# Tokens pass through the experts in four groups of 384 instead of three groups of 512

## The reference

```python
# 1. chunked attention over 2 x 8 heads, 768 positions, head size 64, 8 memory keys
for c in range(24):                                  # chunks of 32 queries
    k_full = concat(mem_k, k[c*32-16 : c*32+40])     # at most 64 keys
    a = softmax(scale * q_c @ k_full.T)              # + 1e-9 in the denominator
    out[c] = a @ v_full
x = out.reshape(1536, 512)

# 2. first mixture: 4 experts, gates given
p = domain_probs / (domain_probs.sum(-1) + 1e-9)
x = sum(p[:, e:e+1] * (relu(x @ w1[e]) @ w2[e]) for e in range(4))   # 512 -> 1024 -> 512

# 3. second mixture: 8 experts, gates from the tokens
P = exp(x @ w_gate - max)
for _ in range(8):
    P /= P.sum(1); P /= P.sum(0); P *= 1536 / 8
out = sum(P[:, e:e+1] * (relu(x @ w1[e]) @ w2[e]) for e in range(8))
```

## Time and profile before

| | |
|---|---|
| time, median of 3 executions | 1686.27 us (1685.75 to 1688.09) |
| span of the profiled execution, first to last instruction | 1684.4 us |
| own time of the profiled execution | not listed apart from its span |
| PE busy | 1651.6 us, 98% of the span |
| DVE busy | 489.4 us, 29% |
| ACT busy | 322.8 us, 19% |
| POOL busy | 35.3 us, 2% |
| share of PE in the chain that ended last | 94% |

### The profile page before, as it was taken

How to read it: one execution, slowest core, us unless ns; L and a number is a source line. 1 busy time by engine, 2 the same in 40 slices (tenths; PEclk the granted TensorE clock), 3 DMA queues, 4 the chain that set the end, 5 groups by cost and what they waited for, 6 DMA issues and landing times.

```text
span 1684.4 us, 19145 instructions
## 1 busy us (share of the span) xinstructions
PE 1651.6 (98%) x8037; PEld 1363.8 (81%) x8037; DVE 489.4 (29%) x811; ACT 322.8 (19%) x551; POOL 35.3 (2%) x39
## 2 busy tenths in 40 slices
PE   6799999999999999999999999999999999999999
PEld 5778888888888887888888888888888888888887
DVE  5541321231231242272132132123123123123212
ACT  4631221121121131121121121112112112112110
POOL 2310000000000000000000000000000000000000
PEclk9799999999999999999999999999999999999999
DMA  8950020020020011002002002002002001100001
GB/s 188 147 167 1 0 100 1 1 100 0 0 99 0 0 50 51 1 3 98 1 0 100 0 0 100 0 0 100 0 0 99 0 0 59 40 0 0 8 17 50
DMA packets 50964, 66.56 MB, mean 40 GB/s; under 512 B 27880, under 2 KB 27880, under 8 KB 50928
## 3 DMA queue, kind: packets, MB, share of 16 engines
q1 hardware_dynamic: 50928, 66.04, 13.5%
HBM read 62.89 MB, written 3.15 MB: 39 GB/s over the span
## 4 chain that ended last, share of the span: by engine, by line
PE 94%; SPq 3%; issue 1%; DVE 1%; ACT 0%; DMA 0%; POOL 0%; POOLq 0%
PE banks L356 31%; PE banks L355 31%; PE banks L357 31%; SPq L187 1%; SPq L186 1%; PE banks L435 0%; DMA v_bd<-in_mem_v 0%; SPq L193 0%; SPq L189 0%; PE banks L316 0%; DVE acc L755 0%; PE banks L406 0%; PE banks L408 0%; PE banks L395 0%; SPq L169 0%
## 5 line engine op out<-in xcount | busy, mean ns | idle before, releaser
L706 DVE SCALAR_TENSOR_TENSOR h_lo<-banks,h_hi 128x512 fp32r<-128x512 f32 x288 | 199.0, 691 | 1130.0 <-ACT h_hi L571 1130.0
L356 PE MATMUL banks<-w_hi,h_hi 128*128 128x512 f32 x1152 | 453.8, 394 | 0.0
L355 PE MATMUL banks<-w_lo,h_hi 128*128 128x512 f32 x1152 | 451.9, 392 | 1.4 <-DVE x_lo L714 1.4
L355 PE MATMUL banks<-x_lo,w_hi 128*128 128x512 f32 x1152 | 448.8, 390 | 0.2
L356 PE MATMUL banks<-x_hi,w_hi 128*128 128x512 f32 x1152 | 448.2, 389 | 0.0
L357 PE MATMUL banks<-x_hi,w_lo 128*128 128x512 f32 x1152 | 447.9, 389 | 0.0
L357 PE MATMUL banks<-w_hi,h_lo 128*128 128x512 f32 x1152 | 447.4, 388 | 0.0
L571 ACT ACTIVATE h_hi<-banks 128x512 fp32r<-128x512 f32 x288 | 171.9, 597 | 1300.7 <-PE banks L357 1300.7
L355 PEld LDWEIGHTS banks<-w_lo,h_hi 128*128 128x128 f32 x1152 | 216.3, 188 | 50.9 <-DVE x_lo L714 1.8
L357 PEld LDWEIGHTS banks<-w_hi,h_lo 128*128 128x128 f32 x1152 | 216.2, 188 | 48.3
L355 PEld LDWEIGHTS banks<-x_lo,w_hi 128*128 128x128 f32 x1152 | 216.2, 188 | 47.3 <-DVE x_lo L744 0.7
(11 more groups left out here) (82 smaller groups left out, 297.4 us busy)
## 6 DMA issues: line engine op xcount, KB each, us to landing
w_raw<-in_moe_w SPq DMA_DIRECT2D x24, 2048.0 KB, 8.1
v_bd<-in_v SPq DMA_DIRECT2D x16, 308.0 KB
w_raw<-in_q SPq DMA_DIRECT2D x8, 384.0 KB, 5.0
w_raw<-in_k SPq DMA_DIRECT2D x8, 384.0 KB
out_x<-acc SPq DMA_DIRECT2D x12, 256.0 KB, 2.1
v_bd<-in_mem_v SPq DMA_DIRECT2D x16, 48.0 KB
v_bd<-in_v SPq DMA_DIRECT2D x16, 10.0 KB
v_bd<-in_v SPq DMA_DIRECT2D x16, 12.0 KB
```

What stands on the lines that cost most here:

```text
L355: pe.matmul(out_, lhs_hi, rhs_lo, start=start, stop=False)
L356: pe.matmul(out_, lhs_hi, rhs_hi, start=False, stop=False)
L706: dve.scalar_tensor_tensor(out=h_lo[:, f % 4, :], in0=h_ps[f % 4], scalar=0.0, in1=h_hi[:, f % 4, :].bitcast(F32), op0=ALU.max, op1=ALU.su ...
```

## The change

`GT` goes from 4 to 3 and `G` from 3 to 4. What follows from it:

- `up` streams 384 columns instead of 512, and there are 32 slots in an expert instead of 24. `down` has 9 matmuls instead of 12, each still 512 wide.
- `h_ps` holds 384 of its bank's 512 columns, and only three of the four `y_ps` are used.
- There is a fourth group to transpose between the mixtures. It is turned right behind the third, at g = 0, f = 4 of the expert 4, and uses the same four banks, so it waits for `x2_part` of the third.
- In the expert 4 the outputs of group 2 are now added with the gate during group 3, and so DVE waits for the scaling and for the zeroed `acc` there instead of behind the expert. The last group, in which the next weights are split, is no longer the one in which the rounds of normalising run.

```diff
-    GT = 4
+    GT = 3
     G = TILES // GT
     GW = GT * P
...
-        h_ps = [banks[i // 2][:, (i % 2) * 512:(i % 2) * 512 + 512] for i in range(4)]
+        h_ps = [banks[i // 2][:, (i % 2) * 512:(i % 2) * 512 + GW] for i in range(4)]
         y_ps = [banks[2 + i // 2][:, (i % 2) * 512:(i % 2) * 512 + 512] for i in range(4)]
...
                 pe.wait_ge(y_taken, GT + ((EA - 1) * G + g + 1) * GT)
                 for c in range(DC):
-                    if g == 1:
-                        pe.wait_ge(x2_lo_ready, c + 1)
+                    if g == 1 or g == 3:
+                        pe.wait_ge(x2_lo_ready, (g - 1) * DC + c + 1)
...
-                pe.wait_ge(h_lo_ready, EA * G * FC + FC - GT + g + 1)
+                pe.wait_ge(h_lo_ready, EA * G * FC + FC - 4 + g + 1)
...
                     if g == 0 and f == 4:
                         turn_x2(2)
+                        turn_x2(3)
...
                     if g == 0:
-                        pe.wait_ge(x2_lo_ready, DC + f + 1)
+                        pe.wait_ge(x2_lo_ready, (DC if f < 4 else 2 * DC) + f + 1)
...
                         if between and g == 0 and f == 4:
-                            for i in range(2 * DC, 3 * DC):
+                            for i in range(2 * DC, 4 * DC):
                                 x2_part(i)
...
                         if f == 1 and g:
-                            accumulate(e, g - 1, plain=between)
+                            if between and g == 3:
+                                dve.wait_ge(rescaled, 2 * GT)
+                                dve.wait_ge(acc_rezeroed, 1)
+                            accumulate(e, g - 1, plain=between and g < 3)
...
             expert(EA, True, between=True)
-            dve.wait_ge(rescaled, 2 * GT)
-            dve.wait_ge(acc_rezeroed, 1)
```

More of the change, by code:

```diff
@@ L55, in build @@
     LEFTROWS = LEFT // ROWTOK
-    assert KEYS == 64 and 2 * D == P and DC == PAIRS and N == B * S and GW == 512 and G == 3
+    assert KEYS == 64 and 2 * D == P and DC == PAIRS and N == B * S and GW == 384 and G == 4
     with ExitStack() as ctx:
```

## The result

The changed kernel takes 1715.28 us (median of 4 executions, 1713.32 to 1718.41) and the kernel before, in the same comparison, 1687.18 us (1685.75 to 1688.94). The ratio is 1.0166 with a 95% interval of 1.0152 to 1.0181, so the change costs 28 us (26 to 31 by the interval). The forecast was 1704.4 us. The measured time is slower as forecast and inside the range of 1688 to 1724, but 11 us above the point forecast.

The account below looks back on a forecast made before the run. The prediction took PE's matmul count times start distance as the bound. Its terms 15.5 + 0.1 + 1.8 + 0.7 = +18.1 us on 1686.3 gave 1704.4 us, 1.1% slower, with a range of 1688 to 1724 us.

Parts of the forecast that it names:

- What bounds it: Whole kernel: time is the number of matmuls times the distance between their starts, plus the attention ahead of it.
- I take 173.4 ns: Start distance of 384-column float32r matmuls: 160.0 ns of columns plus a fixed 13.4 ns for each matmul.
- the cost by columns: Rival for the up matmuls: the extra 13.4 ns shrinks with the columns, 170.0 ns each; 1689 to 1692 us, chance 0.22.
- +15.5 us: All ups: 4608 matmuls at 173.4 ns instead of 3456 at 226.7 ns, 15.5 us more.
- The logits: Logits matmuls go from 24 to 32, at 177.3 ns each: 5.67 us against 5.53, +0.1 us.
- Between the mixtures: Group turns: the fourth group's first bank is free at 3.5 us, +1.5; other turns give some back, sum +0.7 us.
- The attention's end: Behind the last attend: release 0.75 us earlier, but 2.56 us more up work lies behind it, net +1.8 us.
- PE merely idles longer: Ahead of the last attend: shorter ups only lengthen PE's idle time of 1.39 us before v arrives.
- At nothing: Slots and group turns: evictions, accumulations and normalising rounds stay covered despite 4.14 us slots, adding no time.
- a load that weighs more: Rival for the up matmuls: weight load counts more on short streams, 178 to 188 ns; 1725 to 1772 us, chance 0.10.
- the faster case: Rival for the up matmuls: the 13.4 ns belong to long streams, 384 columns take 162.7 ns; 1655 us, chance 0.05.
- the new wait: Rival: a wait appears in every slot or group, for example 47 turns at 0.3 us, +14, 1718 us; chance 0.05.

Follow-up runs that it names:

- the narrowed kernel: Changed kernel with each down beyond the first group cut to 384 of its 512 output columns, so all expert matmuls have 384: 1525.6 us in one execution.
- the width series: Bare float32r streams without the computation, 96 matmuls of each width: 173.6 ns a matmul at 384 columns, 119.9 at 256, 111.5 at 192.

## Why the prediction was right in direction and low in size

- **What bounds it.** Right. PE's distances set the time in both kernels, and no wait came into the slots (900 of 900 us busy).
- **"I take 173.4 ns."** Right as the cost of each matmul, against the cost by columns (170.0 ns). Bare streams give 173.3 once they have settled, the second half of each `up` 173.3, the logits 173.4.
- **"+15.5 us".** This is the term that was mis-sized. It took one distance for all twelve matmuls of an `up`. They average 175.5 ns, since the first six are 26 ns late in sum behind a `down` of 512 columns: 4608 x 175.5 - 783.5 = +25.2 us. The forecast's own range for the fixed part, 11 to 16 ns, held this average (15.5), and that was luck: nothing in it was about a slow start. In the kernel before every stream of the experts has 512 columns, so its trace couldn't show a step between widths. Why the ups start slowly in the real kernel is open, as said above.
- **The logits, "+0.1".** 5.55 us against 5.53: +0.02. Their distance at 512 columns (5.53 / 24 = 230.4 ns) fell by 57 ns and not by 53.
- **Between the mixtures, "at 3.5 us: +1.5".** 3.52 us. The other two turns took 1.23 and 1.66 us, against 1.67 and 2.01 before. In sum that is +0.7 us, as forecast.
- **The attention's end, "+1.8".** The part that is a fixed sum, 2.56 us less hidden work, is in the 28.5: 15.5 + 2.6 + 0.1 + 0.7 = 18.9, and with 26 ns for each of the 380 ups behind the release, +9.8, it comes to 28.7. The other part, a release 0.75 us earlier, held at the full clock. "PE merely idles longer" was wrong in the profiled execution: the clock also fell, at a cost of 1.6 us. It did not in the narrowed kernel behind 3.15 us, and how often it happens can't be said from one trace of each kernel.
- **At nothing.** Evictions, accumulations, the rounds of normalising and the moved waits cost nothing, as forecast: DVE's and ACT's waits for PE are as long as before.
- **The rivals.** The cost by columns, a load that weighs more and the faster case were all refuted by the width series, and the new wait by the busy time of PE. Of the 28.5 us behind the release, the turns between the mixtures have 0.7; nearly all the rest is the width of the `up`.

No version here beats the kernel before. With 512 moving columns an `up` already fills one of the banks of the kernel's layout, and a narrower one pays its 13 ns more often.

## What to carry to other kernels

Where TensorE is full, count matmuls as well as columns: in float32r each one costs about 13 ns over its columns, so a stream of 384 columns is 2.0% dearer per column than one of 512 (173.4 / 384 against 226.7 / 512), before any step between widths. Read distances position by position and not as a mean, and distrust a single price where the change puts two widths next to each other. A bare stream can show that a cause is sufficient; whether it acts in the kernel is shown only by taking it out there, and here the loss stayed. To size a change of 1% beside a stage that waits for transfers, compare the spans behind a common event of both traces: here two of one kernel and three of the other agreed within 0.05 us, where single executions scatter by 3 us and more.

## What the hardware showed unexpectedly

- A step from 512 to 384 moving columns makes the next six matmuls 26 ns slower in sum (21 ns behind only three matmuls of 512), in streams that wait for nothing. Behind steps from 384 to 512 in the same kernels, 12 matmuls took 2.76 us, where 12 without a step take 2.72.
- In the real kernel the turn from `down` to `up` keeps a loss of about 27 ns when all have 384 columns, and its downs of 512 columns take 229 ns a matmul where bare ones take 226.7. The cause of both is open.
- The fixed part of a float32r matmul isn't quite a constant: 17 ns at 480 columns, 16 at 448 (twice), 15 at 416, 13 at 352, 320, 256 and in long streams of 384, 12 at 288. At 224, 192 and 128 columns the distance stays at 111 to 112 ns. In bfloat16 the fixed part is 2.5 ns at 512, 384, 256 and 128 columns.
- An idle PE of 4.3 us, and one of 2.4 us in another execution, was followed by an attend of 2.5 to 2.7 us instead of 1.54. One of 3.15 us, one of 1.4 and one of 1.0 were not. So the idle time just ahead doesn't alone tell whether the clock falls.
